# Mixture-of-experts stage with stationary weights over blocks of 288 tokens, and a last layer that runs in sorted order

## The reference

```python
# 1: attention, B, H, S, D = 4, 8, 576, 64, with a bias computed from positions
attn = softmax(q @ k.T / sqrt(D) + bias) @ v            # -> x [N=2304, 512]
# 2: mixture of experts, top 1 of E = 8, F = 1024
logits = x @ w_gate; e = argmax(logits)
gate_w = softmax(logits)[e]
out[mask_e] = gate_w[mask_e] * (relu(x[mask_e] @ w1[e]) @ w2[e])
# 3: gated layer, FF = 1536
xn = x / sqrt(mean(x*x) + 1e-6) * rms_g
g = xn @ w_gate
y = (g * sigmoid(g) * (xn @ w_val)) @ w_out             # [2304, 512]
```

## Time and profile before

| what | value |
|---|---|
| median of 3 runs | 1179.83 us (1178.24 to 1179.99) |
| the profiled execution | 1178.37 us, its span 1176.5 us |
| PE busy | 1076.9 us (92%) |
| DVE busy | 711.0 us (60%) |
| ACT busy | 505.5 us (43%) |
| POOL busy | 261.2 us (22%) |

### The profile page before, as it was taken

One profiled execution on the slowest core, in us unless ns is written; L12 is line 12 of the kernel. 1 busy time (PEld: TensorE's weight loads), 2 busy tenths in 40 slices (PEclk: granted clock), 3 DMA queues, 4 the chain that ended last, 5 costly groups with the idle time before them and its releaser, 6 DMA issues. The chain is left out here.

```text
span 1176.5 us, 23238 instructions
## 1 busy us (share of the span) xinstructions
PE 1076.9 (92%) x6472; PEld 902.9 (77%) x6473; DVE 711.0 (60%) x1246; ACT 505.5 (43%) x1040; POOL 261.2 (22%) x214
## 2 busy tenths in 40 slices
PE   3969999999998399999999938999999999999997
PEld 1347777777775287788888828999999999999996
DVE  6955565555653752642522238977768777787765
ACT  4977776777764242633412255323232132222111
POOL 4027465565640110200100043410000000000000
PEclk9989999999999599999999969999999999999999
DMA  5574554735521591551111144010000000100001
GB/s 132 222 277 94 146 139 90 200 81 145 137 60 31 199 356 45 172 196 42 45 44 36 36 127 151 28 28 27 27 27 0 27 27 0 53 0 0 27 1 27
DMA packets 78078, 102.92 MB, mean 87 GB/s; under 512 B 45024, under 2 KB 49120, under 8 KB 78048
## 3 DMA queue, kind: packets, MB, share of 16 engines
q1 hardware_dynamic: 74848, 92.06, 26.0%
q0 software_dynamic: 3200, 10.49, 3.0%
HBM read 75.13 MB, written 27.39 MB: 87 GB/s over the span
## 5 line engine op out<-in xcount | busy, mean ns | idle before, releaser
L1418 DVE RECIPROCAL f_eg<-f_eg 128x384 f32<-128x384 f32 x72 | 183.3, 2546 | 0.0
L562 DVE CUSTOM_DVE_ANT_0 a_sc<-a_s_ps,a_bias 128x576 f32<-128x576 f32 x144 | 108.2, 753 | 86.5 <-PE a_s_ps L478 68.4
L1383 ACT ACTIVATE f_eg<-f_g 128x384 f32<-128x384 f32 x72 | 35.4, 492 | 283.3 <-PE f_v L1453 283.3
L624 ACT ACTIVATE a_pr<-a_sc,a_nmax 128x576 f32<-128x576 f32 x144 | 111.9, 777 | 39.7 <-DVE a_nmax L562 35.0
L478 PE MATMUL a_s_ps<-a_khi,a_qs 128*128 128x288 f32 x320 | 103.4, 339 | 9.7 <-PEq L82 9.0
L1453 PE MATMUL f_g<-f_xhi,f_ghi 128*128 (+1 forms) x288 | 99.5, 346 | 6.6 <-DVE f_eg L1422 3.7
L495 PE MATMUL a_t_ps<-ident,a_pr 128*128 128x128 f32 x720 | 102.4, 272 | 1.3 <-ACT a_pr L624 0.5
L1453 PE MATMUL f_g<-f_xhi,f_glo 128*128 (+1 forms) x288 | 98.3, 341 | 0.0
L1453 PE MATMUL f_g<-f_xlo,f_ghi 128*128 (+1 forms) x288 | 98.2, 341 | 0.0
L1453 PE MATMUL f_v<-f_xhi,f_vhi 128*128 (+1 forms) x288 | 97.6, 339 | 0.0
L1453 PE MATMUL f_v<-f_xlo,f_vhi 128*128 (+1 forms) x288 | 97.6, 339 | 0.0
(11 more groups left out here) (225 smaller groups left out, 2375.8 us busy)
## 6 DMA issues: line engine op xcount, KB each, us to landing
e_raw<-ew SPq DMA_DIRECT2D x20, 1024.0 KB, 7.1
bias_ihj<-b_res SPq DMA_DIRECT2D x36, 288.0 KB, 2.1
a_qraw<-q SPq DMA_DIRECT2D x32, 288.0 KB, 5.1
a_kraw<-k SPq DMA_DIRECT2D x32, 288.0 KB, 5.7
a_bias<-bias_ihj SPq DMA_DIRECT2D x16, 576.0 KB, 6.7
y_sorted<-e_out SPq DMA_DIRECT2D x21, 256.0 KB, 2.0
a_v<-v SPq DMA_DIRECT2D x32, 128.0 KB, 2.3
x_tokens<-a_xp SPq DMA_DIRECT2D x64, 64.0 KB, 1.7
```

The lines of the kernel that those rows point to most:

```text
L562: e.tensor_tensor_reduce(sc[:, h, :].rearrange("p (a s) -> p a s", a=2), s_ps[:, h, :, 0:HALF], bias[:, 2 * s + h, :].rearrange("p (c s) - ...
L624: mm = e.activation(pr[:, w, S * h:S * h + S], sc[:, h, :], ACT.Exp, bias=nmax[:, h:h + 1], scale=-1.0, accum_out=sums[:, u, 2 * s + h:2 * ...
L1383: e.activation(eg[:, k % 2, :], g_ps[k % 2][:, 0:CHUNK], ACT.Exp, scale=-1.0).then_inc(s_e, 1)
L1418: e.reciprocal(x, x).then_inc(s_c, 1)
```

## The change

After attention there is one program block: each engine runs straight from routing through the experts into the last layer, with no meeting in between. The memory of both is laid out by hand in one arena. Experts now take blocks of 288 tokens, so 576, 17, 559, 576 and 576 tokens make 2 + 1 + 2 + 2 + 2 = 9 blocks, where blocks of 128 made 21.

- The weights are stationary and the tokens move: every matmul has 288 columns. Eight steps f per block, each an `inner` (12 matmuls: 128 of the F rows) and, two steps later, an `outer` (12 matmuls, into four PSUM banks that hold the transposed output). The hidden rows come out transposed already, so `turn_h` is gone.
- The weights have one slot; each half is overwritten as soon as its last use in the old expert is over (`SPLITS`).
- The gate weight is applied to the gathered rows (`scale`). For that routing has a second chain of 18 matmuls, which makes `gs`.
- The square sums, the root, the inverse and the norm are made per expert block, on the transposed output, during the next block (`squares_fold`, `squares_sum`, `root`, `inverse`, `normal`). The normed transposed rows go to `xn`, in sorted order and without padding.
- The last layer loads its chunks from `xn` with direct transfers, already transposed; its preparation is one split on ACT and one on DVE. Its outputs go out by indirect transfers from POOL to the tokens' rows.
- The zero fill of the unused rows of `y_sorted` is gone.

```diff
-NBLK = (N + E * (P - 1)) // P
+BT = HALF
+NBLK = (N + E * (BT - 1)) // BT
+SUB, ROWS = (P, P, BT - 2 * P), (P, P, P)
...
+    # ExpertStage
+    SPLITS = {1: 3, 4: 0, 6: 1, 7: 2}
...
+    def turned(self, i, s):
+        return self.banks.x if not isinstance(i, int) or s == 0 else self.banks.h[3 - s]
...
+        def turn(i, s):                                   # PE
+            e.wait_ge(self.s_xs, sem.at(self.s_xs, i * NSUB + s + 1))
+            if not isinstance(i, int):
+                e.wait_ge(self.s_xl, sem.at(self.s_xl, i * NSUB + s))
+                if s == 0:
+                    e.wait_ge(self.s_rt, sem.at(self.s_rt, i - 1))
+            rows, bank = ROWS[s], self.turned(i, s)
+            for k in range(KD):
+                mm = e.transpose(bank[:, k * P:k * P + rows], self.xin[0:rows, s, k * P:(k + 1) * P],
+                                 self.ident[0:rows, 0:rows])
+            mm.then_inc(self.s_xt, 1)
...
+            for f in range(KF):                           # PE, one block
+                if f in (0, 4):
+                    e.wait_ge(ew.s_w, sem.at(ew.s_w, run * 4 + f // 2 + 1))
+                inner(i, u, f)
+                if f == 2:
+                    with e.If(i > 0):
+                        self.squares_sum(e, i)
+                if 3 <= f < 6:
+                    turn(i + 1, f - 3)
+                if f == 2:
+                    e.wait_ge(ew.s_w, sem.at(ew.s_w, run * 4 + 2))
+                    e.wait_ge(self.s_yc, sem.at(self.s_yc, i))
+                if f == 6:
+                    e.wait_ge(ew.s_w, sem.at(ew.s_w, run * 4 + 4))
+                if f >= 2:
+                    outer(i, f - 2)
+            outer(i, 6)
+            outer(i, 7)
...
+            for f in range(KF):                           # ACT, one block
+                e.wait_ge(self.s_h, sem.at(self.s_h, i * KF + f + 1))
+                e.wait_ge(self.s_o, sem.at(self.s_o, i * KF + f - (1, 1, 4, 2, 2, 2, 2, 2)[f]))
+                e.activation(self.hhi[:, f % 3, :], self.banks.h[f % 3][:, 0:BT], ACT.Relu).then_inc(self.s_hh, 1)
+                if f < NSUB:
+                    scale(i + 1, f)
+                if f == 3:
+                    with e.If(i > 0):
+                        self.root(e, i)                   # ACT.Sqrt, needs s_ss
+                if 4 <= f < 7:
+                    x_hi(i + 1, 1 - u, f - 4)
+                if f in self.SPLITS:
+                    split(self.SPLITS[f])
+            e.wait_ge(self.s_yc, sem.at(self.s_yc, i + 1))
+            e.wait_ge(self.s_pre, sem.at(self.s_pre, i))
+            e.activation(self.sq[:, :, :], self.y[:, :, :], ACT.Square).then_inc(self.s_sq, 1)
...
+            for f in range(KF):                           # DVE, one block
+                e.wait_ge(self.s_hh, sem.at(self.s_hh, i * KF + f + 1))
+                e.scalar_tensor_tensor(out=self.hlo[:, f % 3, :], in0=self.banks.h[f % 3][:, 0:BT], scalar=0.0,
+                                       in1=self.hhi[:, f % 3, :].bitcast(f32), op0=ALU.max, op1=ALU.subtract)
+                if f in (0, 3, 4):
+                    with e.If(i > 0):
+                        (self.squares_fold, None, None, self.inverse, self.normal)[f](e, i)
+                if 4 <= f < 7:
+                    x_lo(i + 1, 1 - u, f - 4)
+                if f in self.SPLITS:
+                    split(self.SPLITS[f])
+            e.wait_ge(self.s_o, sem.at(self.s_o, i * KF + KF))
+            e.wait_ge(self.s_st, sem.at(self.s_st, i * self.PER))
+            e.tensor_copy(self.y[:, :, :], self.banks.y[:, :, 0:BT]).then_inc(self.s_yc, 1)
...
+    def squares_fold(self, e, n):                         # DVE: [P, 4, 288] -> [P, 288]
+    def squares_sum(self, e, n):                          # PE: ones x pre -> banks.x
+    def root(self, e, n):                                 # ACT: Sqrt(banks.x)
+    def inverse(self, e, n):                              # DVE: reciprocal [P, 288]
+    def normal(self, e, n):                               # DVE: four [P, 288], in0 * rg * inv
...
+        # RoutingStage.tensor, a second chain
+        e.wait_ge(self.s_g, sem.at(self.s_g, 1))
+        for t in range(NT):
+            mm = e.matmul(banks.y[:, 3, 0:NCOL], self.inq[:, t, :].bitcast(f32), self.inbg[:, t, :], start=(t == 0), stop=(t == NT - 1))
...
+        # FfnStage.sync
+        e.wait_ge(ex.s_st, sem.at(ex.s_st, used * ex.PER - ex.PER))
+        self.load_x(e, 0)
+        e.wait_ge(ex.s_o, sem.at(ex.s_o, used * KF))
+        for n in range(5, 8):
+            self.load(e, n)
+        ex.store(e, used, used - 1)
+        for n in range(8, 12):
+            self.load(e, n)
...
+        # FfnStage.gpsimd: hi and lo of the first five weight pieces and of chunk 0, then the late lo parts, then
+                e.indirect_dma_start(self.out, bass.IndirectOffsetOnAxis(ap=self.cols[:, c * self.TPC + t:c * self.TPC + t + 1], axis=0),
+                                     self.ob[:, t, :], None).then_inc(self.s_st, 16)
...
+            # FfnStage.scalar and .vector, step (0, 0)
+                self.ex.root(e, used)
+                e.activation(self.warm[:, :], self.ex.rt.eps[:, :], ACT.Exp)
...
+                ex.inverse(e, used)
+                ex.normal(e, used)
```

More of the change, by code:

```diff
@@ L417, in pair @@
                     store_second(p - 1, 1 - u)
-            for i in range(NT, NBLK):
-                e.dma_start(ys[i * P:(i + 1) * P, :], zero[:, :]).then_inc(s_zd, 16)
             each_pair(e, pair)
@@ L672, in _, with __init__, at, run @@
                 keep_out(NPAIR - 1, half)
+class Arena:
+    SLAB, HALF_SLAB, RAW, XIN, XPAR, LATE, BYTES = 0, 65536, 131072, 147456, 155648, 167936, 204800
+    def __init__(self, nc, sb):
+        self.nc = nc
+        self.fence = sb("arena", [P, self.BYTES // 4])
+        self.base = nc.sbuf_base - self.BYTES
+    def at(self, name, shape, offset, dtype=f32):
+        return self.nc.alloc_sbuf_tensor_at(name, shape, dtype, offset=self.base + offset)
+    def run(self, offset):
+        state = [offset]
+        def place(name, shape, dtype=f32):
+            n = 4
+            for d in shape[1:]:
+                n *= d
+            here = state[0]
+            state[0] = here + (n + 31) // 32 * 32
+            return self.at(name, shape, here, dtype)
+        return place
+class Banks:
+    def __init__(self, nc, ctx):
+        ps = lambda n, s: ctx.enter_context(nc.psum_tensor(n, s, f32))
+        self.y = ps("m_y", [P, 4, 512])
+        self.h = [ps(f"m_h{i}", [P, 512]) for i in range(3)]
+        self.x = ps("m_x", [P, 512])
 class Routing:
@@ L687, in __init__ @@
         self.start, self.inc = sb("r_start", [P, E + 1]), sb("r_inc", [P, E + 1])
+        self.idx = sb("r_idx", [P, NCOL], i32)
+        self.gs = sb("r_gs", [P, NCOL])
+        self.lead = sb("r_lead", [P, 1], i32)
+        self.tabs = sb("r_tabs", [P, 128], i32)
         self.s_c = sem("r_c")
+        self.s_lead, self.s_idx, self.s_gs, self.s_tab = (sem("r_" + n) for n in ("lead_s", "idx_s", "gs_s", "tab_s"))
     def constants(self, e):
@@ new lines, in __init__, with cut, part, lead @@
+        self.s_hi, self.s_w = sem("e_hi"), sem("e_w")
+    def cut(self, w1, w2, c):
+        h = c // 2
+        return w2[:, 4 * h:4 * h + 4, :] if c % 2 else w1[:, :, 512 * h:512 * h + 512]
+    def part(self, low, c):
+        return self.cut(self.w1[low], self.w2[low], c)
+    def lead(self, c):
+        return self.cut(self.lead1, self.lead2, c)
+    def source(self, c, expert):
+        h, w = c // 2, self.dram[c % 2][bass.ds(expert, 1), :, :, :].rearrange("a p k f -> p (a k) f")
+        return w[:, 4 * h:4 * h + 4, :] if c % 2 else w[:, :, 512 * h:512 * h + 512]
```

1318 lines of the change are left out of this document (647 added, 671 removed).

## The result

The changed kernel takes 1280.4 us (median of 4 runs, 1278.1 to 1282.6) against 1179.9 for the kernel before: a ratio of 1.0855, 95% interval 1.0832 to 1.0878. It is slower, as predicted, but by 100 us, not by 28; the time lies 50 us above the top of the range. The profiled execution has a span of 1276.3 us.

What follows compares the result with a forecast made beforehand. Time was set by PE's expert matmuls, whatever holds PE there, and two holes. 1178.4 + 5 (start) + 48 (experts) + 6 (clock) − 23 (hole) − 6 − 2 + 1 (last layer, outputs) = 1207.4, forecast 1208 us, range 1186 to 1230.

Steps and rivals of the forecast that it cites:

- Start of the experts: Routing's extra work for `gs` delays the first expert matmul to 411.5 to 416.5 from 409.6: +5 us.
- PE's work in a block: Matmuls, remaining transposes and sum over partitions of one expert block: 26.7 us if nothing held PE.
- The waits of the turning: PE waits per block at f = 5 (2.0 us), f = 4 (3.6) and f = 3 for the root (2.44 with load).
- The hole: Gap between experts and last layer goes, its first chunk being ready in time: −23 us, bound −18.
- f = 2, "0.4 us": PE's wait for `squares_sum` in each block: its inputs need 5.1 us against three `inner` of 1.56.
- The clock, "+6 us": Half clock after PE's long waits in expert blocks: 0.8 us each, +6 us, bounds 0 and 27.
- the clock swings: Rival: each block's holes bring half clock after two of them, 27 us in place of 6; 1220 to 1250, chance 0.14.
- The weight splits, "nothing": Splits at f = 1, 4, 6, 7 hide behind PE's work; costed at nothing, up to 2 us per switch.
- The drain of 1.38 us: The skill's drain at each table switch, 11 us in all; left out of the sum because the trace shows none.

Runs made afterwards that it cites:

- square_later: Changed kernel with ACT's Square of a block moved from the block's end to behind Relu(0) of the next block; 1257.1 us.
- no_root: Changed kernel with ACT's Sqrt left out; DVE multiplies the sum by 1/512 and takes the larger of that and 1 before its reciprocal; 1248.9 us.
- sum3: The order kernel with the sum over partitions (`squares_sum`) one step of f later, behind `inner` of f = 3; 1178.9 us.
- fill: Changed kernel with useless matmuls of 288 columns put into PE's waits at f = 2 (26 of them), 3, 4 and 5; 1273.8 us.
- fill_short: The fill kernel with 8 instead of 26 useless matmuls at f = 2; 1264.3 us.
- turn_later: Changed kernel with the three turnings of the next block's rows one step of f later, behind `inner` of f = 4, 5, 6; 1228.4 us.
- order: Changed kernel with both the turnings one step of f later and Square behind Relu(0) of the next block; 1203.6 us.
- cand2: sum3 with weight splits at f = 2, 4, 6, 7, norm behind the split of x, last layer's first chunk loaded early, token numbers on their own semaphore; 1169.3 us.

## Why the prediction was wrong in size

Right were the direction, the mechanism of the turning (turning and root held PE behind work that starts only after its own last group) and these terms:

- Start of the experts: first matmul at 415.5 (forecast 414.6, range 411.5 to 416.5). Block 0 from there to its copy 32.6 us, forecast 35.3 with the slow start.
- PE's work in a block, 26.7 us; matmuls 0.132 us apart (forecast 0.130).
- The waits of the turning: f = 5 1.80 (2.0), f = 4 3.40 (3.6), root 2.40 (2.44), every root with its load (9 of 9).
- The hole: 23 us became 2.65, since POOL's split of the first chunk ended late; the bound of −18 covered it.

Three terms of the sum were mis-sized:

1. **f = 2, "0.4 us".** Measured 4.2 us a block on average (33.4 / 8), 30 us too little in the sum. Missing in all eight blocks were ACT's change of block (0.96 or 1.38 us), a second table load, the one in front of Relu(0), and 0.8 us of the fold. The second load should have been in the sum: I gave each Sqrt its load and the function behind it none, though the earlier trace rows show both (722.81 and 727.05). The change of block could only be bounded. The fold was priced by the slope of plain operations; this one reads its 1152 inputs across the tile. That Square, the change of block and the load sit in PE's wait is shown by square_later (−16 us by place alone), no_root (0.9 to 1.3 us less in each plain block without the load) and sum3 (nothing left with one group more ahead). The fold's 0.8 us is read from the timeline alone.
2. **The clock, "+6 us".** The half clock in the experts is 32.7 us, 1.3 of it in block 0: 31 in the other eight, over my bound of 27 and 25 more than the 6 of the sum. The rival "the clock swings" had the right mechanism with a chance of 0.14. I argued against it that the holes of 2.0 and 3.6 us were shorter than the 3.75 seen before; but after the wait of 3.40 the clock stayed at 0.50 for over 5 us, where the earlier trace rows have some 3. The missed wait at f = 2 added the second dip. fill and fill_short show that the waits cause it. The trace agrees with the Trainium skill, TensorE: Matmul & The Clock Gate, section "A second HAM failure mode: psum-queue depth-cycling", on the swing between bursts; here it costs 9% of the expert stage (32.7 of 381).
3. **The weight splits, "nothing".** I gave them up to 2 us for each of 4 switches, "if they surface", and left them out. Two surfaced, with 3.2 and 1.6 us: they are 4.8 of the 33.4 us above. In the faster kernels this became the longest wait once the others were out (turn_later, order, sum3).

By block: 43.5 us (from the copy at 448.15 to the one at 796.30, eight blocks) against 35.9. Of the 7.6 between, 3.8 are the fold's wait (0.6 of it the weights), 3.1 the clock, and the rest the two passes of `squares_sum` (0.75 us at full clock, forecast 0.3) and 0.4 of matmul pace, less 0.4 by which the turning's two waits were shorter than forecast. Eight blocks: 61 us, less 3 for block 0: the stage is 381 us where the sum had 322.

The other 12 us lie behind: 2.7 in the gap; 6 in the last layer (469.2 for 463.2), where the first chunk's outputs come 97.7 us after its first matmul (799.10 to 896.79, forecast 90.9) while later chunks are faster than forecast (75.2 for about 76); 8.0 us behind the last matmul instead of 5.9; and 0.9 at the start. In the first chunk PE waits 5.0 us (up to 813.2) for a first Exp that stands behind the root and its two table loads, and the norm's four operations take 4.2 us beside POOL's splits; no kernel was run that separates these.

The drain of 1.38 us that the Trainium skill, ScalarE: Activation LUTs, section "What ACT_TABLE_LOAD costs", puts on a load is not seen: Relu starts 0.01 us behind its load (583.01), and the gap ahead of it is as long in no_root, where there is no load.

## What to carry to other kernels

When a function switch enters a loop, count a load on both sides, and ask which chain the second one stands in. A block's chain also pays the change of block on each engine: put work that others wait for behind the first operation of the new block, not at the end of the old. Price a repeated wait of 3 us of PE as wait plus clock, here a third on top (32.7 on 97.8). And such a change can be lost by its order alone: three moved steps took 1280 us to 1179. Each removed wait then showed a transfer that it had covered, and room for those gave 1162. Look for that transfer in the slow kernel already: it was in two of its eight waits at f = 2.

## What the runs showed of the hardware

- Loads stand in front of Relu too: 14 at L1228. Two of them are in block 0 (418.86 and 427.27), where no Sqrt has run yet. Later blocks have one at Relu(0), and every second block one at Relu(4) as well; its next load at Relu(0) comes with no Sqrt in between (511.18 and 540.86). So a load doesn't depend on what ran last. That it follows from the program's text, the loop of two blocks and its conditions, fits these places and is not shown by a run.
- Beside POOL's splits some operations of DVE take far longer, others not. In cand2 the norm of the last block falls beside them (POOL runs from 671.26 on with pauses of at most 0.1 us): four operations take 10.24 us instead of 1.80. The ones behind them, which read a bank of PSUM, take their usual 0.45 and 0.68, though POOL runs from 681.72 to 685.26. No run takes the splits away, so that POOL is the cause is argued from this.

```profile
671.71 10.24 DVE L1269 SCALAR_TENSOR_TENSOR e_y<-e_y,f_rg,e_inv 128x288 f32<-128x288 f32 x4
681.88 0.45 DVE L1303 SCALAR_TENSOR_TENSOR e_hlo<-m_h,e_hhi 128x288 fp32r<-128x288 f32 x1
682.24 0.68 DVE L1278 TENSOR_TENSOR e_xlo<-m_x,e_xhi 128x512 fp32r<-128x512 f32 x1
```

- The fold, a reduction of 1152 elements to 288 across the tile, takes 2.13 us, a copy of 1152 elements 1.36.
